# A three-stage kernel on one core: VectorE's softmax steps set inside its g steps, and the opening reordered

## The reference

```python
def _attn_ref(x, state):                      # x (8, 8, 512, 64), state (8, 8, 32, 64)
    scores = scale * np.matmul(x, state.transpose(0, 1, 3, 2))
    scores = scores - scores.max(-1, keepdims=True)
    a = np.exp(scores)
    a /= a.sum(-1, keepdims=True) + 1e-09
    xread = np.matmul(a, state)
    scores2 = scale * np.matmul(state, x.transpose(0, 1, 3, 2))
    scores2 = scores2 - scores2.max(-1, keepdims=True)
    a2 = np.exp(scores2)
    a2 /= a2.sum(-1, keepdims=True) + 1e-09
    sread = np.matmul(a2, x)
    return np.concatenate([xread, sread], axis=2)

def _moe_ref(x, w_in, w_out):                 # x (4352, 512), w_in (512, 2048)
    h = x @ w_in
    g = np.maximum(0.01 * h, h)
    return g @ w_out

def _moe2_ref(x, w_gate, w_output_gate, w1, w2):   # 8 experts, top 1
    logits = x @ w_gate
    e_idx = np.argmax(logits, axis=1)
    gate_w = softmax(logits)[np.arange(N), e_idx]
    eom = 1.0 / (1.0 + np.exp(-(x @ w_output_gate)))
    for e in range(E):
        mask = e_idx == e
        out[mask] = gate_w * eom[mask, e] * (np.maximum(x[mask] @ w1[e], 0.0) @ w2[e])
```

## Time and profile before

| | us |
|---|---|
| runs shown | 1175.81, 1176.22, 1174.80 (median 1175.81) |
| the profiled execution, its own time | 1174.99 |
| its span, first to last instruction | 1173.2 |
| PE busy | 1127.1 (96% of the span) |
| PE loading weights | 918.9 (78%) |
| DVE busy | 596.5 (51%) |
| ACT busy | 401.1 (34%) |
| POOL busy | 151.1 (13%) |
| DMA, mean | 67 GB/s |

### The profile page before, as it was taken

One profiled execution on the slowest core, in us unless ns is written; L12 is line 12 of the kernel. 1 busy time (PEld: TensorE's weight loads), 2 busy tenths in 40 slices (PEclk: granted clock), 3 DMA queues, 4 the chain that ended last, 5 costly groups with the idle time before them and its releaser, 6 DMA issues.

```text
span 1173.2 us, 18305 instructions
## 1 busy us (share of the span) xinstructions
PE 1127.1 (96%) x6690; PEld 918.9 (78%) x6691; DVE 596.5 (51%) x1310; ACT 401.1 (34%) x752; POOL 151.1 (13%) x195
## 2 busy tenths in 40 slices
PE   5999999999999999999999999999999999999995
PEld 2677777777777777777777888899989989889884
DVE  6575474664754754746645576542322225265221
ACT  3344334334434333343343454311211214153211
POOL 1000001010010010010100202312121223233221
PEclk9999999999999999999999999999999999999998
DMA  9211120120120211200101401651111112442110
GB/s 353 104 51 37 37 77 1 39 75 1 41 73 1 77 38 36 77 1 1 37 1 36 163 35 26 208 188 54 36 54 36 54 52 66 170 149 81 38 43 30
DMA packets 38398, 78.44 MB, mean 67 GB/s; under 512 B 9255, under 2 KB 10535, under 8 KB 38312
## 3 DMA queue, kind: packets, MB, share of 16 engines
q1 hardware_dynamic: 29221, 52.92, 12.9%
q0 software_dynamic: 9120, 24.76, 6.6%
HBM read 59.75 MB, written 20.61 MB: 69 GB/s over the span
## 4 chain that ended last, share of the span: by engine, by line
PE 80%; DVE 12%; ACT 3%; issue 3%; DMA 1%; POOL 0%; DVEq 0%; ACTq 0%; SPq 0%; POOLq 0%
PE bank L491 24%; PE bank L493 23%; PE bank L492 23%; PE bank L524 2%; DVE g_buf L1125 2%; DVE gT_lo L1127 1%; ACT gT_hi L912 1%; PE bank L746 1%; PE bank L542 1%; PE bank L558 1%; DVE a_buf L1079 1%; DVE v_lo L1119 1%; DVE small L1078 1%; DVE a_buf L1067 1%; DVE small L1055 1%
## 5 line engine op out<-in xcount | busy, mean ns | idle before, releaser
L491 PE MATMUL bank<-wout_lo,gT_hi 128*128 128x512 f32 x544 | 215.6, 396 | 0.0
L493 PE MATMUL bank<-wout_hi,gT_hi 128*128 128x512 f32 x544 | 212.2, 390 | 0.0
L492 PE MATMUL bank<-wout_hi,gT_lo 128*128 128x512 f32 x544 | 212.0, 390 | 0.0
L1125 DVE TENSOR_TENSOR g_buf<-g_buf,bank 128x512 f32<-128x512 f32 (+1 forms) x144 | 94.2, 654 | 105.7 <-ACT g_buf L906 105.4
L491 PE MATMUL bank<-xgT_lo,w_hi 128*128 128x256 f32 x512 | 145.3, 284 | 1.9 <-DVE w_lo L1242 1.1
L493 PE MATMUL bank<-xgT_hi,w_hi 128*128 128x256 f32 x512 | 144.9, 283 | 0.0
L492 PE MATMUL bank<-xgT_hi,w_lo 128*128 128x256 f32 x512 | 144.9, 283 | 0.0
L1127 DVE TENSOR_TENSOR gT_lo<-g_buf,gT_hi 128x512 fp32r<-128x512 f32 (+1 forms) x144 | 95.4, 663 | 95.4 <-ACT gT_hi L912 95.4
L912 ACT CAST gT_hi<-g_buf 128x512 fp32r<-128x512 f32 (+1 forms) x144 | 85.9, 597 | 138.9 <-DVE g_buf L1125 138.9
L906 ACT ACTIVATE g_buf<-bank 128x512 f32<-128x512 f32 (+1 forms) x144 | 82.6, 573 | 145.0 <-PE bank L493 144.1
L997 ACT ACTIVATE hT_hi<-bank 128x256 fp32r<-128x256 f32 x128 | 48.9, 383 | 237.5 <-PE bank L493 226.8
(11 more groups left out here) (210 smaller groups left out, 1696.8 us busy)
## 6 DMA issues: line engine op xcount, KB each, us to landing
raw<-w_dram SPq DMA_DIRECT2D x20, 1024.0 KB
rows_dram<-y_buf SPq DMA_DIRECT2D x8, 1032.0 KB
X<-x_in_dram SPq DMA_DIRECT2D x8, 1024.0 KB, 5.4
XT<-xT_in_dram SPq DMA_DIRECT2D x7, 1024.0 KB, 5.2
win<-w_in_dram SPq DMA_DIRECT2D x4, 1024.0 KB, 11.9
y_buf<-w_out_dram POOLq DMA_DIRECT2D x6, 512.0 KB, 7.3
XT<-xT_in_dram SPq DMA_DIRECT2D x2, 512.0 KB, 4.6
stT<-stT_in_dram SPq DMA_DIRECT2D x8, 128.0 KB, 2.2
```

Source lines behind the costliest of these rows:

```text
L491: pe.matmul(o, l_hi, r_lo, start=first, stop=False)
L492: pe.matmul(o, l_lo, r_hi, start=False, stop=False)
L493: return pe.matmul(o, l_hi, r_hi, start=False, stop=last)
L1125: dve.tensor_tensor(g_buf[:, n, 0:w], g_buf[:, n, 0:w], up_b[n][:, 0:w], ALU.max).then_inc(g_ready, 1)
```

## The change

It has four parts.

1. **Steps set between the two halves of a g step.** A new function `beside_g` on DVE is called between the maximum and the `gT_lo` subtraction of step `f` in layers 0 to 6: `norm_T(a, 0)` at 8, `max_rows(a, 1)` at 9, `turn_rows(a, 0)` at 10, `turn_rows(a, 1)` at 11, `a_lo(a, 0)` at 13. They stood after the subtraction of the same step, except `turn_rows(a, 1)`, which stood at step 12. `norm_rows(a, 1)` moves from after step 11's g step to after step 10's, ahead of `v_rest(b, 3)`. On ACT, `a_hi(a, 1)` moves from step 13 to 12.
2. **The opening's maximum by halves.** `max_half` takes the maximum and subtracts it for 256 tokens, so the first half needn't wait for the second. `exp_rows` of the opening still does all 512 and now waits for both semaphores, `half_shifted` and `sc_shifted`.
3. **States times W_in early.** `make_v(0, 1)`, its `keep_v` and its `v_rest` move from step 2 of layer 0 to the opening; the product goes to banks `acc[0:2]`, which hold the first half of the scores until it has been transposed.
4. **The first `up`.** `first_up` does the six matmuls of `up(0, 0)` in another order, each pair behind its own wait: hi by hi, then those with `aT_lo`, last those with `v_lo`. DVE does `a_lo` ahead of `v_rest(0, 0)`.

```diff
@@ first_up, on PE
+            def first_up():
+                o, cols = up_b[0][:, :], slice(0, P)
+                pe.wait_ge(v_hi_done, 2)
+                for g in range(2):
+                    pe.wait_ge(aT_hi_done, g + 1)
+                    pe.matmul(o, v_hi[0][:, g, cols], aT_hi[0][:, g, :], start=(g == 0), stop=False)
+                for g in range(2):
+                    pe.wait_ge(aT_lo_done, g + 1)
+                    pe.matmul(o, v_hi[0][:, g, cols], aT_lo[0][:, g, :], start=False, stop=False)
+                for g in range(2):
+                    pe.wait_ge(v_lo_done, v_count(0, 0, g))
+                    last = pe.matmul(o, v_lo[0][:, g, cols], aT_hi[0][:, g, :], start=False, stop=(g == 1))
+                last.then_inc(up_done, 1)
@@ the end of PE's opening
             scores_T(0)
+            pe.wait_ge(half_turned, 2)
+            make_v(0, 1, to=acc[0:2])
@@ beside_down, step 2
-                if f == 2 and b < B:
-                    if r is not None:
-                        pe.wait_ge(yT_ready, 4 * r + 2)
-                    else:
-                        pe.wait_ge(exp2_done, 2)
+                if f == 2 and 0 < b < B:
+                    pe.wait_ge(yT_ready, 4 * r + 2)
                     make_v(b, 1)
@@ exp_rows, on ACT
+                if a == 0:
+                    act.wait_ge(half_shifted, p + 1)
                 act.wait_ge(sc_shifted, 2 * a + p + 1)
@@ a layer and the opening, on ACT
-                        elif f == 13:
+                        elif f == 12:
                             a_hi(a, 1)
             split_piece(0)
+            keep_v(0, 1, of=acc[0:2])
             exp_T(0, 0)
@@ max_half, on DVE
+            def max_half(g, half):
+                dve.wait_ge(half_turned, 2 * half + g + 1)
+                s3 = a_buf[:, g, half_toks(half)].rearrange("p (h n) -> p h n", n=NS)
+                top8 = max1[g][:, 8 * half:8 * half + 8]
+                step = Steps(dve, att_step, 2 * half + g, 1)
+                step(dve.reduce_max(top8, s3, AX.X))
+                dve.tensor_tensor(s3, s3, top8.rearrange("p (h o) -> p h o", o=1).broadcast_to([P, 8, NS]),
+                                  ALU.subtract).then_inc(sc_shifted if half else half_shifted, 1)
@@ beside_g and the g step, on DVE
+            def beside_g(a, f):
+                if f == 8:
+                    norm_T(a, 0)
+                elif f == 9:
+                    max_rows(a, 1)
+                elif f == 10:
+                    turn_rows(a, 0)
+                elif f == 11:
+                    turn_rows(a, 1)
+                elif f == 13:
+                    a_lo(a, 0)
                 dve.tensor_tensor(g_buf[:, n, 0:w], g_buf[:, n, 0:w], up_b[n][:, 0:w], ALU.max).then_inc(g_ready, 1)
+                if b < B - 1:
+                    beside_g(b + 1, f)
                 dve.wait_ge(g_hi_done, u)
@@ a layer, on DVE
                         elif f == 8:
-                            norm_T(a, 0)
                             norm_T(a, 1)
                             max_rows(a, 0)
                         elif f == 9:
-                            max_rows(a, 1)
                             norm_rows(a, 0)
                         elif f == 10:
-                            turn_rows(a, 0)
+                            norm_rows(a, 1)
                     if b < B and f in (2, 6, 10):
                         v_rest(b, (f + 2) // 4)
-                    if a is not None and f == 11:
-                        norm_rows(a, 1)
                         if f == 12:
-                            turn_rows(a, 1)
                             keep_a2(a, 0, aux[0])
@@ the opening, on DVE
-            turn_half(0, 0)
-            turn_half(1, 0)
-            turn_half(0, 1).then_inc(sc_turned, 1)
-            max_rows(0, 0)
-            turn_half(1, 1).then_inc(sc_turned, 1)
-            max_rows(0, 1)
+            for half in range(2):
+                for g in range(2):
+                    turn_half(g, half)
+                for g in range(2):
+                    max_half(g, half)
             norm_rows(0, 0)
             turn_rows(0, 0)
             norm_rows(0, 1)
             turn_rows(0, 1)
-            v_rest(0, 0, of=acc[2:4])
             a_lo(0, 0)
             a_lo(0, 1)
+            v_rest(0, 0, of=acc[2:4])
             max_T(0, 0)
             max_T(0, 1)
             split_piece(0)
+            v_rest(0, 1, of=acc[0:2])
```

37 lines of the change are left out of this document (21 added, 16 removed).

## The result

| | before | changed |
|---|---|---|
| median of 4 runs, us | 1175.55 (1174.80 to 1176.22) | 1160.93 (1160.78 to 1161.36) |
| ratio | 1 | 0.9876 (95% interval 0.9859 to 0.9894) |
| the profiled execution | 1174.99 | 1160.88 |
| its span | 1173.2 | 1158.7 |

The change takes 14.6 us off the median; the forecast was 13.4.

The account below looks back on a forecast made before the run. PE, busy 96%, was taken to bound the kernel, losing time to waits for DVE's order. Part 1's 12.4 us plus the opening's 1.0 made 13.4 off, forecasting 1162.4 us against the median; range with opening rivals 1158.8 to 1166.5.

Parts of the forecast that it names:

- The waits in the layers: PE's waits for the flip and v_lo come from DVE's order; removing them gains 11.1 us in six layers, 1.3 in layer 0.
- `norm_rows`' 1.82 us: Layers, DVE: norm_rows ahead of v_rest gives back 1.82 us there and brings rank_read 2.1 us earlier for the flip.
- The halves cancel against the table load: Opening: the 1.28 us load falls behind the wait for sc_shifted, so halves bring nothing; without the misplaced load, 1.1 us.
- The rival by the rule of the Trainium skill: Opening loses: 1.4 us of drain behind the table load delays all that follows; 1163.8 to 1164.7, chance 0.10.
- The opening, 1.0 forecast: Opening up to down(0, 1), parts 3 and 4: 1.0 us gained, the middle between clock bounds of 0.1 and 2.2.
- matmul starts 0.44 apart until about 28: Opening, PE: the low clock, with matmuls 0.44 us apart, was expected to last until about 28.
- the prediction's own list of signs that it is wrong: Longer v_lo waits, a wait ending late elsewhere in the same layers, or 0.23 us spacing before 26 or after 30.5.
- my upper bound: Opening: if the clock rises at 26, as if the pause didn't count, down(0, 1) starts at 31.3, gaining 2.2 us.
- what is late next: Check for new waits: step 9's later subtraction is covered by 4.1 us, and read_states and the keep_a2 pair gain none.
- The opening gives more: Rival, opening: the clock rises early (2.2) or the table load doesn't hold DVE up (1.1 more); 1160.1, chance 0.12.
- The wait only moves: Rival, layers: gaps save half, 1.05 us, so up(b, 12) waits 0.77 longer for v_rest; 1169.3, chance 0.05.
- Slower: Rival, layers: gap work and ACT's cast stretch each other, up(b, 12) waits 2.1 us more in seven layers; 1179.4, chance 0.03.

Follow-up runs that it names:

- e3: The changed kernel with norm_rows(a, 1) back behind step 11, turn_rows(a, 1) in step 12 and a_hi(a, 1) in step 13; 1159.64 us, ratio 0.9865.
- e4: The changed kernel without part 1: the new opening with the old order of steps in layers 0 to 6; 1174.18 us, ratio 0.9988.
- e5: The changed kernel with a one-column exponential added ahead of exp_rows, so that the table load comes at the start; 1159.44 us, ratio 0.9862.
- e10: The changed kernel run again with no edit, for a second profile of its opening; 1161.27 us, ratio 0.9875.
- e1: The kernel before with part 1 alone, its opening left as it was; 1162.77 us, ratio 0.9890.
- e2: The kernel before with only norm_rows(a, 1) moved ahead of v_rest(b, 3), nothing set in the gaps; 1183.27 us, ratio 1.0073.
- e6: The changed kernel with v_rest(0, 1) between the halves of the first g step instead of ahead of it; 1159.74 us, ratio 0.9866.
- e8: The changed kernel with early table load, norm_rows(a, 1) back at step 11, v_rest(0, 1) and layer 0's own steps in gaps; 1155.89 us, ratio 0.9837.

## Why the prediction was right

**The waits in the layers** were read rightly. "Issue" was DVE's routing: e3, with only the gaps of the steps ahead of it filled, takes that wait off PE's list, and e4, without them, has it back. The gaps between the halves take the steps at unchanged durations. 1.85 us a layer were forecast, 1.96 measured; the row of layer 1 gives 1.54 for the flip, as priced, and 0.35 instead of 0.3 for `up(b, 12)`. Layer 0 gave 1.54, not 1.3. These small misses make 0.9 of the 1.2 us by which the gain was under-forecast. The lower end of the range, 1158.8, doesn't follow from the terms named for it: 1162.4 - 1.2 - 0.7 - 1.1 is 1159.4. Nothing hangs on it.

**One step of the reasoning was redundant.** I let `norm_rows`' 1.82 us pay for the flip and counted its cost at `v_rest`. The order is right, but e3 shows that the gaps alone pay for both waits, and the move loses 0.2 us a layer.

**The halves cancel against the table load**, to within 0.15 us (4.97 and 4.79 against 4.83). The rival by the rule of the Trainium skill (ScalarE: Activation LUTs, "What ACT_TABLE_LOAD costs"), 1.38 us of drain with each switch of the set, falls. With a drain behind the load the exponential of the changed kernel would start at 13.7, and it starts at 12.30, right where the load ends. Ahead of the load there is none either: it starts 0.09 us after the end of the subtraction that it waits for (10.50 + 0.42 on DVE). The page's figure for the load itself agrees with the row. The 1.1 us that the prediction gives to halves without the misplaced load are 1.3 in e5.

**The opening, 1.0 forecast and 1.24 measured, was right in size by luck and wrong in working.** The size itself is loose: the second half started 0.68 us later than in the profile before, so counted from there the gain is 1.92 us, and in the second profile (e10) it is 1.46, or 0.26 from the start of the program. The failing step is the one on the clock: "matmul starts 0.44 apart until about 28", from "the rise came some 6 us after PE began to work without a pause". With the old opening the first rise came at 25.9 in one profile and at 23.1 in another (e1), so the 6 us aren't a constant. In the changed kernel `make_v(0, 1)` gives PE work at 15.24, and behind it, at 16.79, a matmul already takes 0.50 us and not the 0.76 or more of the low level; then the clock falls at 19.8, behind a wait of 1.56 us that I hadn't listed (the second matmul of `first_up`, for the second cast of `aT_hi`; with the early load of e5 it waits 0.42), and is up again at 23.2. A distance of 0.23 us before 26 was on the prediction's own list of signs that it is wrong, and it stands there: 25.68, 25.91, 26.14. The pause of 1.57 us that I priced was forecast at 1.5 and did happen, but no fall of the clock came behind it in this execution. So `down(0, 1)` gained 2.12, near my upper bound of 2.2, and 2.80 counted from the second half. The second failing step is what is late next: `read_states(0)` had 0.18 us of wait for `keep_a2` before, and I didn't follow DVE's chain in layer 0 to steps 3 and 4. There `split_piece(2)` and the maximum of step 4 stand between the two copies, so PE, 2.12 earlier, lost 0.86 of that again. The Trainium skill (TensorE: Matmul & The Clock Gate, "Part 1: The HAM clock gate") has the clock follow how busy PE has recently been. The rows agree that it falls in or behind waits and rises behind work, but they don't give a length of wait from which it does.

**The rivals.** "The opening gives more" held for the clock's half (2.12) and not for the load's; e5 shows what the load's half would have been. "The wait only moves" is refuted for the gaps by e1, whose six layers are 11.7 us shorter; e2 shows that it is just what the move of `norm_rows` does by itself. "Slower" is refuted: DVE's and ACT's instructions last what they did (L1128 0.70, L1176 0.69; ACT's cast has a mean of 597 ns on both pages). e2 is the slower kernel that this rival described, a wait for `v_lo` in seven layers, but of 2.1 us in each and with nothing in the gaps; and four falls of the clock (layer 0's and three more) lie on top of it, which no rival had.

**What stays open** is when the clock falls. Once it had risen, it read 0.50 in or behind single waits of 1.22 us (e6, the second matmul of `first_up`), 1.52, 1.56, 1.91, 1.93, 1.97, 2.17, 2.30 and 2.68 us, and in three of e2's six layers with 1.61 and 0.47. It stayed at 1.00 behind 0.41 (e8), 1.21 (e3, `up(0, 2)`), 1.57 (changed, `up(0, 2)`), 1.61 (e4, `make_v(0, 1)`), 1.66 (e2, the first flip) and 1.78 (e8), in the other three layers, and at each of the twelve flips of before and e4 that waited 1.38 to 1.44. The length of the wait alone doesn't decide it, and no run here isolates what does.
